# Gathered rows of the first network: turned in 32x32 squares by VectorE and moved between tiles by DMAs from ScalarE's queue, in place of TensorE transposes

## The reference, cut to what matters

```python
q, k, v, alpha: (4, 8, 768, 48)                       # decayed linear attention
state = alpha[:, :, t, :, None] * state + k_t v_t^T;  y[:, :, t] = q_t @ state
x = y rearranged to (3072, 384)                       # N tokens, D features
# first network: E = 8 experts, F = 1024, each token goes to its best expert
expert_idx = argmax(normalised x @ normalised emb.T / tau);  gate = softmax(logits)[expert_idx]
for e in range(8):
    h = relu(x[mask_e] @ w1[e]);  out[mask_e] = gate * (h @ w2[e])
# second network, dense, 384 -> 2048 -> 384
h = out @ w_in;  result = max(0.01 * h, h) @ w_out
```

## Time and profile before

| what | value |
|---|---|
| median of 3 runs | 803.26 us (802.3 to 806.18) |
| profiled execution | 803.95 us, its span 802.2 us |
| TensorE busy | 791.6 us, 99% of the span |
| VectorE, ScalarE, GpSimd busy | 456.6, 340.6, 207.3 us |
| TensorE's share of the chain that ended last | 93% |
| stretch 200 to 360 us | TensorE 160.0 of 160 us, VectorE 103.6, ScalarE 77.9, GpSimd 54.9, DMA engines 0.72 |

### The profile page before, as it was taken

How to read it: one execution, slowest core, us unless ns; L and a number is a source line. 1 busy time by engine, 2 the same in 40 slices (tenths; PEclk the granted TensorE clock), 3 DMA queues, 4 the chain that set the end, 5 groups by cost and what they waited for, 6 DMA issues and landing times.

```text
span 802.2 us, 17151 instructions
## 1 busy us (share of the span) xinstructions
PE 791.6 (99%) x5025; PEld 689.1 (86%) x5026; DVE 456.6 (57%) x721; ACT 340.6 (42%) x625; POOL 207.3 (26%) x281
## 2 busy tenths in 40 slices
PE   8999999999999999999999999999999999999998
PEld 7888888889989989989888888888888888888987
DVE  7899987686567476575565343433534433434332
ACT  3554544566446256444344334324323332433323
POOL 6666632223333342331132003001200400100100
PEclk9999998999999999999999999999999999999999
DMA  9997764666774766976640212203202102100301
GB/s 227 273 264 237 223 221 135 237 172 189 259 236 149 245 174 195 288 207 191 155 46 2 39 30 90 39 1 108 50 0 78 40 0 64 55 1 23 96 1 40
DMA packets 74610, 101.84 MB, mean 127 GB/s; under 512 B 35783, under 2 KB 59891, under 8 KB 74560
## 3 DMA queue, kind: packets, MB, share of 16 engines
q1 hardware_dynamic: 65312, 86.13, 37.6%
q0 software_dynamic: 5952, 15.04, 6.1%
q10 hardware_dynamic: 3296, 0.06, 0.2%
HBM read 67.82 MB, written 19.58 MB: 109 GB/s over the span
## 4 chain that ended last, share of the span: by engine, by line
PE 93%; DMA 3%; DVE 1%; issue 1%; POOL 1%; DVEq 0%; ACT 0%; SPq 0%; ACTq 0%; POOLq 0%
PE bank L1813 24%; PE bank L1874 20%; PE bank L1786 16%; PE bank L1766 15%; PE bank L1864 4%; PE bank L1594 3%; PE bank L1632 3%; DMA qkas<-qka 2%; PE bank L1611 2%; PE bank L1640 1%; PE bank L1742 1%; PE bank L1600 1%; PE bank L1585 1%; PE bank L1652 1%; POOL kt L721 0%
## 5 line engine op out<-in xcount | busy, mean ns | idle before, releaser
L1813 PE MATMUL bank<-yT,wts 128*128 128x512 f32 x864 | 204.8, 390 | 0.3 <-DVE g L1368 0.3
L1813 PEld LDWEIGHTS bank<-yT,wts 128*128 128x128 f32 x864 | 161.9, 188 | 34.4 <-DVE g L1368 0.7
L1874 PE MATMUL bank<-gs,wts 128*128 128x512 f32 x720 | 169.7, 389 | 0.0
L1874 PEld LDWEIGHTS bank<-gs,wts 128*128 128x128 f32 x720 | 135.2, 188 | 28.0
L1368 DVE TENSOR_TENSOR g<-bank,small 128x512 f32<-128x512 f32 x96 | 66.0, 687 | 148.8 <-ACT small L975 148.8
L1766 PE MATMUL bank<-wts,gxT 128*128 (+1 forms) x549 | 133.6, 396 | 0.1
L975 ACT ACTIVATE small<-bank 128x512 f32<-128x512 f32 x96 | 57.2, 596 | 166.6 <-PE bank L1813 163.0
L1766 PEld LDWEIGHTS bank<-wts,gxT 128*128 128x128 f32 x549 | 100.8, 188 | 20.8 <-issue 0.7
L1560 DVE TENSOR_TENSOR gs<-g,gs 128x512 fp32r<-128x512 f32 x96 | 66.5, 693 | 66.8 <-ACT gs L1081 66.4
L1081 ACT ACTIVATE gs<-g 128x512 fp32r<-128x512 f32 x96 | 60.8, 633 | 86.0 <-DVE g L1368 84.2
L823 POOL DMA_INDIRECT out<-os,tokens x20 | 19.7, 986 | 291.3 <-ACT os L1070 286.7
(11 more groups left out here) (190 smaller groups left out, 838.4 us busy)
## 6 DMA issues: line engine op xcount, KB each, us to landing
raw<-weights SPq DMA_DIRECT2D x60, 512.0 KB, 4.9
hds<-hs SPq DMA_DIRECT2D x116, 128.0 KB, 3.0
qkas<-qka SPq DMA_DIRECT2D x20, 675.5 KB, 5.7
vs<-v SPq DMA_DIRECT2D x24, 192.0 KB, 4.3
x_rows<-xs SPq DMA_DIRECT2D x24, 192.0 KB, 3.9
yl<-y_rows SPq DMA_DIRECT2D x20, 192.0 KB, 4.3
x_rows<-raw SPq DMA_DIRECT2D x20, 192.0 KB, 3.2
os<-x_rows SPq DMA_DIRECT2D x5, 768.0 KB, 4.5
```

The costliest lines, as they stand in the source:

```text
L1813: m = pe.matmul(gps[f % 2][:, :], wts[:, 0, w_part, n:n + P], yT[:, 1 - u, y_part, k], start=(k == 0 and (w_part, y_part) == (0, 0)), stop ...
L1874: m = pe.matmul(out_turned[u][k][:, :], wts[:, 1, w_part, n:n + P], gs[:, f % 4, g_part], start=(f == 0 and (w_part, g_part) == (0, 0)), s ...
```

## The change

For the blocks from 6 on (25 of 31), TensorE's transposes go. VectorE turns the gathered rows in 32x32 squares from `xg` to a new tile `xq` (`turn_x`, one instruction of 128x384), ScalarE issues four DMAs that move the bands of partitions to a second tile `xd` (`move_x`), and `gx_round` and `gx_rest` read `xd` in SBUF instead of the PSUM bank. In the loop, VectorE turns block w+6 in step w, ahead of `copy_ys` of w; ScalarE moves block w+5 in step w, between `relu` and what follows it. GpSimd's gather waits for the squares of the block two before instead of the TensorE transposes. `xq` and `xd` lie in memory that the second network uses later. The rows of w1 are ordered anew on the host, and the transposes that stay (blocks 0 to 5) read every third column. VectorE's loop is two steps shorter, and two more are written out.

```diff
+        SQUARED = 6
+        def x_passed(w, u):
+            return (w * 8 - 8 * (SQUARED - 2) - 8 * u) * QUADS
+        def x_square(ap):
+            return ap.rearrange("p (k i t) -> p k i t", i=QUADS, t=SQ)
+        def x_in_place(u):
+            return xd[:, u].rearrange("p (i k t) -> p k i t", i=QUADS, t=SQ)
+        def squared(w):
+            return not isinstance(w, int) or w >= SQUARED
...
+            def rows_read(w):
+                if squared(w):
+                    pool.wait_ge(x_squared, w - SQUARED + 1)
+                else:
+                    pool.wait_ge(gx_turned, w + 1)
...
-                        pool.wait_ge(gx_turned, first_gather + n - 1)
+                        rows_read(first_gather + n - 2)
...
             def gx_round(w, u):
-                act.wait_ge(gx_turned, w + 1)
-                act.activation(gxT[:, u, 0], gxps, ACT.Copy).then_inc(gx_hi, 1)
+                if not squared(w):
+                    act.wait_ge(gx_turned, w + 1)
+                    act.activation(gxT[:, u, 0], gxps, ACT.Copy).then_inc(gx_hi, 1)
+                    return
+                act.wait_ge(x_moved[u], x_passed(w, u))
+                act.wait_ge(h_ready, w * 2 - 2)
+                act.activation(x_square(gxT[:, u, 0]), x_in_place(u), ACT.Copy).then_inc(gx_hi, 1)
+
+            def move_x(w, u):
+                act.wait_ge(x_squared, w - SQUARED + 1)
+                for i in range(QUADS):
+                    act.dma_start(xd[:, u, i * PIECE:(i + 1) * PIECE], xq[i * SQ:(i + 1) * SQ, u]).then_inc(x_moved[u], 16)
...
                     for half in range(2):
                         relu(block, at, half)
+                    if squared(block + 2) and ahead(block, 2):
+                        move_x(block + 2, at)
...
+            def turn_x(w, u):
+                dve.wait_ge(gathered[u], w // 2 * 16 + 16 if isinstance(w, int) else w * 8 + (16 - 8 * u))
+                if not (isinstance(w, int) and w < SQUARED + 2):
+                    dve.wait_ge(x_moved[u], x_passed(w, u) - 16 * QUADS)
+                dve.transpose(xq[:, u].rearrange("p (n f) -> p n f", f=SQ),
+                              xg[:, u].rearrange("p (f n) -> p n f", f=SQ)).then_inc(x_squared, 1)
...
                 if not (isinstance(w, int) and w == 0):
+                    later = w + 5 if isinstance(w, int) and w < CLOSE else w + 6
+                    if ahead(later, 0):
+                        turn_x(later, of(w, 1 - u, later))
                     copy_ys(w, u)
...
-            each_window(dve, step)
+            each_window(dve, step, 7)
...
-                    m = pe.transpose(gxps[:, k * P:(k + 1) * P], xg[:, u, k * P:(k + 1) * P], ident[:, :])
+                    m = pe.transpose(gxps[:, k * P:(k + 1) * P], xg[:, u, k::KD], ident[:, :])
...
-                    if rows_first(w) and ahead(block, 1):
+                    if rows_first(w) and ahead(block, 1) and not squared(block + 1):
                         turn_gx(block + 1, 1 - at)
```

More of the change, by code:

```diff
@@ L310, in build @@
         gx_turned = sem("gx_turned")
+        x_squared = sem("x_squared")
+        x_moved = [sem(f"x_moved{j}") for j in range(2)]
         gx_hi = sem("gx_hi")
@@ L1493, in step @@
                         gx_rest(block + 1, 1 - at)
+                    elif isinstance(w, int) and block == SQUARED:
+                        turn_x(block + 2, at)
                     if isinstance(w, int) and block == w + 2:
@@ L1953 @@
     E, D, F = moe_w1.shape
-    w1 = moe_w1[:, features].reshape(E, D // 128, 128, F).transpose(0, 2, 1, 3).reshape(E, 1, 128, -1)
+    w1 = moe_w1[:, features].reshape(E, 1, 128, -1)
     w2 = moe_w2.reshape(E, 4, F // 128, 32, D).transpose(0, 3, 1, 2, 4).reshape(E, 1, 128, -1)
```

14 lines of the change are left out of this document (11 added, 3 removed).

## The result

The changed kernel takes 827.28 us (median of 4 runs, 826.76 to 830.81) against 804.11 us for the kernel before (4 runs, 802.3 to 806.18). The ratio is 1.0309, with an interval of 1.0287 to 1.0332: 3.1% slower, where 817 us (1.7% slower) was forecast. (The two medians alone divide to 1.0288. All ratios and intervals here are those on record for the repeated runs, and can differ from a quotient of medians by some 0.2%.) The profiled execution has a span of 825.4 us against 802.2.

A forecast was written before the change was run, and what follows sets the result against it. The prediction took TensorE to bound the kernel, busy for 99% of the span. 803.95 - 6.1 (transposes) + 18.7 (circle) + 1.2 (start) = 817.75, 0.7 lower for the median: 817 us, 1.7% slower, range 799 to 828.

The forecast's parts named there:

- the deciding term: The circle of VectorE's wait, copy, GpSimd's scatter and next gather: 18.7 us of waits of TensorE.
- What leaves TensorE: Transposes ahead of the hidden layer in 25 blocks, 0.245 us each from start to start: 6.1 us saved.
- The circle: VectorE's gather wait delays copy, scatter and next gather; a turn is 4.2 us plus landing, against TensorE's 8.39: 18.7 us.
- L: The landing time of a gather in the circle, 5.5 us on average; over 4.2 us the circle is slower than TensorE.
- the lengthening: Moves of gathered rows add transfers, which speaks for longer gather landings; a mean of 6.1 us gives 824.
- the shortening: VectorE's turn_h and SyncE's loads get earlier, which speaks for shorter gather landings; a mean of 4.9 us gives 810.
- Its second place on the Trainium skill: DMAs of several engines share 16 DMA engines, so ScalarE's queue wins issue time alone and new moves lengthen gather landings.
- ScalarE's issues: Four DMA issues per block, 2.2 to 2.4 us a step; 0 to 1 us per step with both halves, otherwise nothing.
- The squares: VectorE's 128x384 transpose per block: 0.6 us with semaphore, upper bound 1.1 because it reads with a step of 12 elements.
- the slow transpose: Rival: squares take 1.1 instead of 0.6 us in every turn, 10.5 us more, 827.5; chance 0.07 for this or worse.
- ScalarE's issues are only cost: Case added to the no-change rival: ScalarE's issues alone cost time; 799.4 to 803.4 us, chance 0.18 together.
- the case of no change: Rival: landings shrink to near 3.1 us and the circle hides; 799.4 to 803.4 us, chance 0.18.

The follow-up runs named there:

- e4: The kernel before with TensorE's transposes of the blocks from 6 on left out and nothing in their place: 795.3 us, ratio 0.9902.
- e13: The changed kernel with gathers one step earlier; roundings of gathered rows read a fixed tile and wait for no move, all moves still made: 809.21 us.
- e14: As e13, but with the gathers where the changed kernel has them, not one step earlier: 828.67 us, ratio 1.0295.
- e18: As e13, but without ScalarE's four issues of moves: 798.54 us, ratio 0.994.
- e1: The changed kernel with VectorE's copy to ys put ahead of the squares of the gathered rows: 825.92 us, ratio 1.0281.
- e19: As e13, with the same 100 issues but a quarter of each move's packets and bytes: 806.77 us, ratio 1.0054.
- e15: As e12, but the squares read 32 neighbouring features: 808.42 us, ratio 1.0063.
- e11: As e9, but the squares read 32 neighbouring features: 862.96 us, ratio 1.0761.
- e3: The changed kernel, but the squares read 32 neighbouring features instead of every twelfth: 826.5 us, ratio 1.0282.
- e12: As e9, but VectorE makes the squares of block w+6 ahead of turn_h: 811.87 us, ratio 1.0097.
- e16: As e12 from step 4 on, with the changed kernel's order of moves up to there: 805.31 us, ratio 1.003.
- e9: The changed kernel with gathers one step earlier and ScalarE issuing block w+6's moves as the last thing of step w: 869.27 us, ratio 1.083.
- e7: The changed kernel with SyncE, not ScalarE, issuing the moves of the gathered rows, ahead of its loads: 833.71 us, ratio 1.0377.
- e8: As e7, with the gathers one step earlier: 835.54 us, ratio 1.0382.

## Why the prediction was right and wrong

The direction and the deciding term held; the size fell 10 us short, 24.8 us slower against 13.7. Term by term, forecast against runs:

- **What leaves TensorE**, 25 x 0.245 = 6.1 us: 7.9 by e4 (5.6 to 10.2 by its interval), 0.34 per block by the timelines, 8.5 in all. The interval doesn't exclude 6.1; the timelines do, since the start-to-start distance left out the 0.1 us by which the hidden layer's matmuls got shorter.
- **The circle**, 18.7 us of waits of TensorE: 17.3 us of time by e13 to e14. Right in mechanism; in size partly by luck. The two profiled executions lie 21.1 us apart. Between them TensorE's waits from 150 to 420 us grow by 12.8 us (10.2 to 23.0), not by 18.7, and another 8 us are what matmuls at the lower clock took longer, which the sum didn't have (below).

  The waits also lie elsewhere in part: in the kernel after 12.9 us stand behind the low part of the hidden rows, where about 19 were named, and 7.0 behind that of the gathered rows, where the prediction named none (3.1 of it at the start, which e13 and e18 have too). The last contraction ends 22.9 us later (409.9 and 432.8 us), where 14 was named; what follows keeps its length, as forecast.

  VectorE's squares waited 41.4 us for gathers where some 40 were named, and the copy to `ys` came 7 us late where 4 to 8 was named. The landings kept their lengths: from 160 to 400 us min/median/max 3.1/4.6/6.9 us against 3.1/4.9/7.0 before, so neither the lengthening nor the shortening that the prediction weighed came. (Its second place on the Trainium skill has the moves lengthen L "as the forecast has it"; the sum itself used the landings of before, and these held.) What e1 showed is that it isn't the copy alone that closes the circle. GpSimd's next gather also waits for the squares that free `xg` (38.1 us there), which the prediction had left out.
- **ScalarE's issues**, "0 to 1 us for each step with both halves and nothing for the others", 1.2 us with the start: 9 us by e18 to e19, up to 11 with the bytes. This is the step that failed. The duration of an issue was nearly right (median 626 ns against 564 to 598); the cover was not. Room was worked out for one step without splits and one with both halves, from the kernel before, and for issues that start at once. But the issues also wait for VectorE's squares at their head (267.28 to 273.49 above), and ScalarE stood idle behind them in 25 places of the kernel after: 2.1 us on average before splits (up to 4.4), 3.1 before hidden roundings (up to 5.2).
- **The squares**, 0.6 us each: 0.87, with 1.1 as the bound. The row of 128x512 in the earlier trace rows reads neighbouring elements, and this one doesn't. By the Trainium skill ("SBUF — State Buffer", "Door 1: The DMA port swizzle") each new 16-byte line costs, and the trace agrees in sign: 0.87 strided, 0.57 dense. The stride was worth 2.7 us in e15, 6.3 in e11 and 2.1 in e3, of which the intervals tell none clearly from nothing. The squares' whole price is, with the early gathers, in the 3.1 us from e4 to e18. These lie mostly at the start: in e18 TensorE is busy 160.00 of 160 us from 200 on, and waits 3.1 us once, behind the gathered rows.
- **The clock** was not in the sum. The granted clock before was 1.00 from 160 to 360 us. In the kernel after, 24 or 18 matmuls behind a wait took 5.8 to 6.0 us instead of 4.3 five times (the two above and at 269.0, 306.6 and 388.7), 8 us in all. The granted clock was 0.72 there from 269 to 275 us and 0.76 in the stretches of 7 us around the other four: the lower level (1.2 GHz) for a part of the time instead of 2.4 GHz throughout. It belongs to the price of waits, and is within the 17.3 us: e14 has four such groups, 8 us in all, and was granted 0.91 from 160 to 200 us and 0.98 from 200 to 360; e13 has none and was granted 1.00 in both. Not every long wait brings it. In the kernel after, at a granted clock of 1.00:

```profile
363.45 4.43 PE L1842 MATMUL bank<-wts,hT_even 128*128 x24 [2.12 <-DVE hT_even L1507]
```

With the runs' terms the sum is 803.3 - 7.9 + 3.1 + 11.2 + 17.3 + 1.1 = 828.1, the measured ratio times 803.3. The last term closes the sum by construction; the others are each a difference of two kernels whose own intervals are 1.8 to 4.4 us to each side. They were taken off in one order: what late gathers cost without the issues, and what the issues cost beside late gathers, was not measured, so the split between 11.2 and 17.3 holds for this order alone.

Of the rivals, the slow transpose came true in part in the instruction (0.87, not 1.1) and not visibly in the time: its 10.5 us for 0.5 more would be 5.7 for the 0.27 that came, and e3 took the stride away and gained 2.1, which its interval doesn't tell from none. "ScalarE's issues are only cost" was put into the case of no change, at 799 to 803 us; measured alone, with early gathers (e13), they make 809. The rule that I cited from the Trainium skill ("DMA: Bandwidth & Descriptors", "Issuing engines are not separate DMA queues") says that another issuing engine saves only the sequencer's time, "which is usually small relative to the DMA itself". Here it was not small: the four issues took 2.5 to 3.7 us, and the moves landed 2.0 to 7.6 us after them. For the kernel's time the issuing was the larger part, 9 us against the 2.1 that three quarters of the bytes cost.

Open is how e1 splits its 22.6 us between the gathers it still waits for and ScalarE's side, and what part of the 3.1 us of e18 is the squares and what the early gathers. A feature order that the dense squares and TensorE's remaining transposes can share was not found; e12 to e15 suggests that it would be worth some 3 us, about what e16 lacks.

## What to carry to other kernels

A DMA that an engine issues is work of that engine. Four issues of 0.6 us ahead of work that two other engines wait for cost about as much as the transposes that they replaced had (9 us against 8), so ask for each moved issue what it waits for at its head and what stands behind it. When a step gets a new wait, follow the circle through every engine's order until it closes, landings included, and compare its length with the step of the bounding engine. There can be several of like length, and cutting one shows little until the others are cut. To tell waiting from work, keep the work and let its result go unread: that one kernel (e13, with e14, e18 and e19) told apart what nine rearrangements had left open.

## What the runs showed of the hardware

- A 32x32 squares transpose of 128x384 on VectorE takes 572 to 578 ns (medians of e3, e11 and e15) with neighbouring elements and 870 to 879 ns (e9, after, e12) with a step of 48 bytes, 1.5 times.
- Taking away the three transposes ahead of the hidden layer shortens TensorE's step by 0.34 us (8.63 to 8.29, e4), 0.1 more than the gap between their start and the next matmul.
- An issue of one of these moves takes its engine about 0.6 us: on ScalarE a median of 632 ns for 128 rows of 384 bytes (e13) and 613 for 32 (e19), on SyncE 603 for 128 (e7, e8). Single ones take up to 1.9 us (e13).
- After waits of TensorE of 1.9 to 3.3 us the granted clock fell in some cases (after, e14) and not in others. A wait of 3.14 us at 177 us was followed by 5.82 us for 18 matmuls in the kernel after (granted clock 0.76 from 177 to 184 us), and by 4.35 us in e13 (1.00 in the same stretch):

```profile
177.62 4.35 PE L1827 MATMUL bank<-wts,gxT 128*128 x18 [3.14 <-DVE gxT L1371]
```
